# Attention and two MLPs in one kernel: the half tile of keys in the value product, high and low parts stacked on 128 partitions

## The chip, the cores and the metric

The kernel runs on one core of one Trainium2 chip. The metric is the device time of one execution in microseconds (us). All inputs and outputs are float32. Matrix products are made in the format fp32r, in which one pass of TensorE doesn't keep all the bits of a float32. So each float32 operand is split in two: a high part (the value rounded to fp32r) and a low part (the value minus its high part), and the products of the parts are added up in PSUM.

## The reference, cut to what matters

```
q, k, v: (4, 8, 576, 64)            # batch, heads, sequence, head dimension
q_rot, k_rot = rotate(q), rotate(k)
scores = matmul(q_rot, k_rot.T) / sqrt(64)
scores = scores - max(scores)       # over the keys
attn = exp(scores)
attn = attn / (sum(attn) + 1e-9)
x = matmul(attn, v)                 # the value product
x = x as (2304 tokens, 512)
x = (s * relu(x @ w_in)**2 + b) @ w_out       # first MLP, 512 -> 2048 -> 512
h = x @ w2_in
out = (h * sigmoid(1.702 * h)) @ w2_out       # second MLP
```

The change touches the last line of the attention, `matmul(attn, v)`.

## The kernel before

The 32 heads are worked off in 16 pairs, p = 0 to 15; the heads of a pair are h = 0 and h = 1. A head has 576 keys and 576 queries: four full tiles of 128 (NM = 4) and half a tile of 64 (TAIL = 64). The half tiles of the two heads of a pair share 128 partitions: the 64 keys of head 0 lie on partitions 0 to 63, those of head 1 on 64 to 127.

For each pair the kernel does these jobs, under short names that the prediction uses:

- **S** (TensorE, line 627; ST, line 642, for the half tiles): scores of one tile of 128 queries against all 576 keys, eight S jobs and one ST per pair.
- **max** (VectorE, lines 861 and 867) reads a score tile from PSUM and writes the negated row maximum; **exp** (ScalarE, lines 762 and 769) writes the exponentials E to SBUF, with an accumulator read behind each.
- **X, XQ, XT** (TensorE, lines 653, 663, 675 to 679): transposes, after which the keys lie on the partitions. XT makes the half tiles of keys of both heads, 128 partitions by 640 columns.
- **hi, hiQ, hiT** (ScalarE, lines 776, 781, 786) copy the transposed exponentials out of PSUM as high parts; **lo, loQ, loT** (VectorE, lines 871, 875, 879) subtract these from PSUM and leave the low parts. hiT and loT are for the half tiles of keys; each is one instruction of 128 partitions by 640 columns per pair.
- **V, vlo** (GpSimd, lines 540 and 544) split the value rows in a high and a low part, which stand side by side as the 128 stationary columns. The half tile of value rows is loaded on the 64 partitions of its own head, and the other 64 were set to zero once at the start (line 520), so that the keys of the other head count nothing.
- **PV0, PV1** (TensorE, line 699): the value product of head 0 and head 1. Over the five key tiles, the high and the low part of the exponentials pass in turn against the same stationary values. The output of 576 columns crosses a bank of PSUM, so a tile is done in two pieces (256 and 320 columns); the half tile of head 1 is done in three (256, 256 and 64), since its columns wrap around.
- **evac** (ScalarE, line 793) and **sum** (VectorE, line 891) copy the two halves of the output partitions out of PSUM (64 partitions by 576 columns each; sum moves its half to the other 64 partitions), and **finish** (GpSimd, lines 574 to 581) adds them and scales the result.
- **qk** and **klo** (lines 837 and 914) make high and low parts of the rotated queries and keys of a later pair from the transposes of **prep** (line 729).
- **icp** (line 798) copies the transposed reciprocals of the sums.

The order of the work is written out by hand, one list per engine. PE_ORDER, ACT_ORDER, DVE_ORDER, POOL_ORDER and SP_ORDER hold what one step of the loop issues, with a number behind @ that tells how many pairs a job is ahead or behind; the lists named FIRST do the start. Within one step the lists give, for the jobs around the change:

```
PE:   ... XQ XT X10 X11 IT X12 X13 S00 PV0 S01 S02 S03 ST S10 S11 S12 X00 X01 S13 PV1 prep0 ...
ACT:  ... evac1 qk0 hi02 qk1 hi03 hiQ hiT icp hi10 hi11 hi12 hi13 evac0 exp00 exp01 exp02 exp03 expT exp10 exp11 ...
DVE:  ... sum1 inv klo0 lo02 klo1 lo03 loQ loT lo10 lo11 lo12 lo13 max00 sum0 max01 max02 max03 maxT max10 ...
```

Jobs in PSUM take turns in its eight banks (SLOTS), and a job waits until the one before it in its banks has been read (`freed`, `read`). PV0 stands in the banks of XT, so it waits for loT twice over: for its operand and for its banks. S01 follows X11 and X13, S03 follows PV0, S10 follows S02, and PV1 follows S11. On SyncE, load_v (lines 465 and 466) issues two transfers per head for the value rows, behind a wait for vlo of the pair before (v_lo).

After pair 15, GpSimd does the last sums and splits for the first MLP, and both MLPs follow on all engines.

Of the kernel before, what the change touches and what calls it, by code (L numbers as in the profile page):

```python
# [10 lines left out]
P = 128  # L11


def need(eng, sem, value):

    if value > 0:
        eng.wait_ge(sem, value)
# [13 lines left out]
def fused_kernel(nc, q, k, v, w1_in, w1_out, w_s, w_b, w2_in, w2_out,  # L31
# [129 lines left out]
    with outer:  # L161
        def sem(name):
            return outer.enter_context(nc.semaphore(name))
# [53 lines left out]

        qk_in = [sem(f"qk_in{i}") for i in range(2)]
        v_in = [sem(f"v_in{i}") for i in range(2)]
        v_cleared = sem("v_cleared")  # L220
        cleared = sem("cleared")
        rot_step = sem("rot_step")
        rotated = sem("rotated")
# [46 lines left out]
        def read(eng, kind, p, h, j):  # L270
            if kind == "S":
                need(eng, exp_done, 2 * NM * p + NM * h + j + 1)
            elif kind == "ST":
                need(eng, expT_done, p + 1)
            elif kind == "X":
                need(eng, et_lo, 2 * NM * p + NM * h + j + 1)
            elif kind == "XQ":
                need(eng, etQ_lo, p + 1)
            elif kind == "XT":
                need(eng, etT_lo, p + 1)  # L280
            elif kind == "IT":
                need(eng, invT_copied, p + 1)
            elif kind == "PV":
                need(eng, evac_done, 2 * p + h + 1)
                need(eng, half_done, 2 * p + h + 1)
            elif kind == "prep":
                need(eng, qk_lo, 2 * p + h + 1)
# [44 lines left out]
        with ExitStack() as ctx:  # L332
# [25 lines left out]
            Xhi = sb("Xhi", [P, 2, NM, S], F32R)  # L358
            Xlo = sb("Xlo", [P, 2, NM, S], F32R)

            XThi = sb("XThi", [P, S + TAIL], F32R)
            XTlo = sb("XTlo", [P, S + TAIL], F32R)

            ET = [sb(f"ET{i}", [P, S + TAIL]) for i in range(2)]
            V = [sb(f"V{i}", [P, NT, 2, D], F32R) for i in range(2)]
# [79 lines left out]
            def attention_sync(sp):  # L445
                def tails(t, p):

                    return t[2 * p:2 * p + 2, MAIN:S, :]

                def load(p, h, _):  # L450

                    wait_rotated(sp, 2 * p - 2 + h)
                    to = group(raw, *HEAD_TILES[h])
                    for w, t in enumerate((q_h, k_h)):
                        sp.dma_start(to[:, w, 0:NM, :], mains(t, 2 * p + h)).then_inc(qk_in[h], 16)
                        if h == 0:
                            sp.dma_start(to[:, w, NM, :], tails(t, p)).then_inc(qk_in[h], 16)

                def load_next(p, h, _):
                    if p > 1:  # L460
                        load(p, h, 0)

                def load_v(p, h, _):
                    need(sp, v_lo, 2 * (p - 1) + h + 1)
                    sp.dma_start(vraw[:, h, 0:NM, :], mains(v_h, 2 * p + h)).then_inc(v_in[h], 16)
                    sp.dma_start(vraw[rows_of(h), h, NM, :], v_h[2 * p + h, MAIN:S, :]).then_inc(v_in[h], 16)

                def load_next_v(p, h, _):
                    if p > 0:
                        load_v(p, h, 0)  # L470


                def q_copies(p, h, _):
                    if p > 0:
                        sp.wait_ge(qk_lo, 2 * p + h + 1)
                        need(sp, s_done, 2 * NM * (p - 2) + NM * (h + 1))
                        need(sp, sT_done, p - 1)
                        at = h * TAIL
                        for part in range(2):
                            sp.dma_start(Q[h][p % 2][rows_of(part), at:at + S].bitcast(F32), QK[h][p % 2][0:D, part, :].bitcast(F32)).then_inc(q_copied[h], 16)  # L480

                def k_copy(p, h, _):
                    if p > 0:
                        sp.wait_ge(q_copied[h], 32 * p)
                        sp.dma_start(QK[h][p % 2][0:D, :, :].bitcast(F32), QK[h][p % 2][D:P, :, :].bitcast(F32)).then_inc(k_copied[h], 16)

                def put_inv(p, _, __):
                    sp.wait_ge(invT_copied, p + 1)
                    need(sp, inv_in[p % 2], 48 * (p // 2))
                    sp.dma_start(inv_dram[p % 2], invT[p % 2][:]).then_inc(inv_out[p % 2], 16)  # L490

                def get_inv(p, _, __):
                    sp.wait_ge(inv_out[p % 2], 16 * (p // 2 + 1))
                    need(sp, x_done, p)
                    flat = inv_dram[p % 2].rearrange("t p -> (t p)")
                    for h, at, a, n in ((0, 0, 0, S), (1, 0, S + TAIL, MAIN), (1, MAIN, S, TAIL)):
                        sp.dma_start(inv_row[rows_of(h), at:at + n],
                                     flat[a:a + n].rearrange("(o q) -> o q", o=1).to_broadcast([D, n])).then_inc(inv_in[p % 2], 16)

                def after(s):  # L500
                    if s in (6, 8):
                        load_win(sp, (6, 8).index(s))

                for w, t in enumerate((q_h, k_h)):
                    sp.dma_start(group(raw_0, 0, NM)[:, w, :, :], mains(t, 0)).then_inc(first_in[w], 16)
                for w, t in enumerate((q_h, k_h)):
                    sp.dma_start(group(raw_0, NM, NM + 1)[:, w, 0, :], tails(t, 0)).then_inc(first_tails_in, 16)
                for w, t in enumerate((q_h, k_h)):
                    sp.dma_start(group(raw_0, NM + 1, TILES)[:, w, :, :], mains(t, 1)).then_inc(first_in[2 + w], 16)
                load(1, 0, 0)  # L510
                load(1, 1, 0)
                sp.wait_ge(v_cleared, 1)
                load_v(0, 0, 0)
                load_v(0, 1, 0)
                sp.dma_start(sb_sb[:, 0:1], w_s.rearrange("(a b) -> a b", a=1).to_broadcast([P, 1])).then_inc(sb_in, 16)
                sp.dma_start(sb_sb[:, 1:2], w_b.rearrange("(a b) -> a b", a=1).to_broadcast([P, 1])).then_inc(sb_in, 16)
                program(SP_FIRST, SP_ORDER, {"load": load_next, "loadv": load_next_v, "qcopy": q_copies, "kcopy": k_copy, "put": put_inv, "get": get_inv}, after)

            def attention_gpsimd(pool):
                pool.memset(vraw[:, :, NM, :], 0.0).then_inc(v_cleared, 1)  # L520
                pool.memset(zero[:], 0.0)
                for i in range(2):
                    pool.memset(Q[0][i][:, S:NT * P].bitcast(F32), 0.0)
# [11 lines left out]
                        rotate(pool, g, byc, bys, rot_step, rotated, g - 2)  # L535

                def hi_V(p, h, _):
                    pool.wait_ge(v_in[h], 32 * (p + 1))
                    need(pool, pv_done, 2 * (p - 1) + h + 1)
                    pool.tensor_tensor(V[h][:, :, h, :], vraw[:, h, :, :], zero[:, :].unsqueeze(2).broadcast_to([P, NT, D]), ALU.add).then_inc(v_hi, 1)  # L540

# [68 lines left out]
            def attention_tensor(pe):  # L610
# [71 lines left out]
                def PV(p, h, _):  # L682
                    pe.wait_ge(v_lo, 2 * p + h + 1)
                    freed(pe, before[("PV", p, h, 0)])
                    pe.wait_ge(et_lo, 2 * NM * p + NM * (h + 1))
                    if h == 0:
                        pe.wait_ge(etQ_lo, p + 1)
                        pe.wait_ge(etT_lo, p + 1)
                    ps, r = banks("PV", p, h), ROW[0]
                    for j in range(NT):  # L690

                        pieces = PIECES[0] if j < NM or h == 0 else (PIECES[0][0], (BANK, r + MAIN, BANK - r), (r + MAIN, r + S, -TAIL))
                        for a, b, c in pieces:
                            for n in range(2):
                                if j < NM:
                                    x = (Xhi, Xlo)[n][:, h, j, c:c + b - a]
                                else:
                                    x = (XThi, XTlo)[n][:, TAIL + c:TAIL + c + b - a]
                                mm = pe.matmul(ps[:, a:b], V[h][:, j, :, :].rearrange("p a d -> p (a d)"), x,  # L699
                                               start=j == 0 and n == 0, stop=j == NM and n == 1, skip_group_check=True)  # L700
                    mm.then_inc(pv_done, 1)

                def rotated_tile(first, end, t, w):
# [43 lines left out]
            def attention_scalar(act):  # L747
# [35 lines left out]
                def hiT(p, _, __):  # L783
                    act.wait_ge(xT_t, p + 1)
                    need(act, pv_done, 2 * p)
                    act.copy(XThi[:], banks("XT", p)[:, ROW[1]:ROW[0] + S]).then_inc(etT_hi, 1)

                def evac(p, h, _):
                    act.wait_ge(pv_done, 2 * p + h + 1)
# [65 lines left out]
            def attention_vector(dve):  # L855
# [19 lines left out]
                    dve.tensor_tensor(Xlo[:, :, :, MAIN:S], by_heads(banks("XQ", p)), Xhi[:, :, :, MAIN:S].bitcast(F32), ALU.subtract).then_inc(etQ_lo, 1)  # L875

                def loT(p, _, __):
                    dve.wait_ge(etT_hi, p + 1)
                    dve.tensor_tensor(XTlo[:], banks("XT", p)[:, ROW[1]:ROW[0] + S], XThi[:].bitcast(F32), ALU.subtract).then_inc(etT_lo, 1)  # L879

                def invert(p, _, __):
                    dve.wait_ge(eps_done, p + 1)
# [523 lines left out]
```

## Time and profile before

| | before |
|---|---|
| median of 3 runs | 1085.67 us (1085.67 to 1087.19) |
| the profiled execution's own time | 1085.56 us |
| span of its profile | 1083.7 us |
| TensorE (PE) matmul busy | 1046.9 us, 97% |
| VectorE (DVE) busy | 733.1 us, 68% |
| ScalarE (ACT) busy | 634.0 us, 59% |
| GpSimd (POOL) busy | 706.8 us, 65% |
| mean granted TensorE clock | 0.995 of full |

The profiled execution takes 1.9 us more than its span, which lies around it. Its own time is 0.1 us below the median of the runs. The attention fills the first 320 us or so; the rest is the MLPs. The shares of busy time are means over both parts, which have different limits; PE's busy time counts each matmul until its modelled end, though the next one starts before that.

### The profile page before, as it was taken

The page shows a single profiled execution, that of the slowest core. Times are in us where ns is not written, and L with a number is a line of the kernel's source. Part 1 is how long each engine was busy: PE and PEld are TensorE (multiplying, and loading weights), DVE is VectorE, ACT ScalarE, POOL GpSimd, SP SyncE. Part 2 cuts the span into 40 slices and gives each one's busy share as a digit, 9 for nine tenths or more (in the row PEclk, how much of TensorE's full clock was granted, in tenths as well). Part 3 has the DMA queues.
Part 4 walks back from the last instruction along what each step waited for, and adds up shares of the span by engine and source line. Part 5 has one row for each costly group of instructions (what it writes and reads, how often), then busy time and mean ns, then how long its engine had stood idle before and what let it go on. Part 6 is the DMA issues. An engine that isn't in the chain of part 4 may idle for free.

```text
span 1083.7 us, 17067 instructions
## 1 busy us (share of the span) xinstructions
PE 1046.9 (97%) x6234; PEld 965.3 (89%) x6234; DVE 733.1 (68%) x874; ACT 634.0 (59%) x1124; POOL 706.8 (65%) x587
## 2 busy tenths in 40 slices
PE   4899999999978999999999999999999999999998
PEld 4899999999967999999999999999898888898987
DVE  6888888888857656766576654865567655854542
ACT  4887878787755445645555544754465445654442
POOL 6878787878679764676466665666656674565430
PEclk9999999999989999999999999999999999999999
DMA  4555455554113221222122212122221412142101
GB/s 112 128 149 152 110 148 142 153 128 124 42 49 98 88 68 59 78 60 78 60 63 73 79 59 78 59 73 64 75 62 54 141 59 78 59 136 59 59 21 58
DMA packets 100613, 93.03 MB, mean 86 GB/s; under 512 B 15652, under 2 KB 78644, under 8 KB 100532
## 3 DMA queue, kind: packets, MB, share of 16 engines
q1 hardware_dynamic: 99408, 90.94, 29.7%
q8 instruction: 50, 0.82, 0.3%
q10 hardware_dynamic: 1124, 1.02, 0.3%
q14 instruction: 31, 0.25, 0.1%
HBM read 69.44 MB, written 4.79 MB: 68 GB/s over the span
## 4 chain that ended last, share of the span: by engine, by line
PE 68%; POOL 1%; DVE 0%; issue 0%
PE psum L1106 37%; PE psum L1078 31%; POOL wout_lo L1033 0%; POOL win_lo L1023 0%; POOL wsum L1007 0%; POOL wsum L1009 0%; POOL wsum L1006 0%; POOL wsum L1011 0%; DVE x_sums L1135 0%; POOL xT L581 0%
## 5 line engine op out<-in xcount | busy, mean ns | idle before, releaser
L1023 POOL TENSOR_TENSOR win_lo<-win_raw,win_hi 128x768 fp32r<-128x768 f32 x48 | 101.0, 2104 | 249.0 <-ACT win_hi L1017 249.0
L1078 PE MATMUL psum<-xc_hi,win_hi 128*128 128x384 f32 x672 | 227.0, 338 | 7.7 <-POOL xc_lo L558 4.0
L1078 PE MATMUL psum<-xc_lo,win_hi 128*128 128x384 f32 x672 | 226.8, 338 | 0.0
L1078 PE MATMUL psum<-xc_hi,win_lo 128*128 128x384 f32 x672 | 226.3, 337 | 0.0
L1078 PEld LDWEIGHTS psum<-xc_hi,win_hi 128*128 128x128 f32 x672 | 127.0, 189 | 17.4 <-POOL xc_lo L558 4.4
L1078 PEld LDWEIGHTS psum<-xc_lo,win_hi 128*128 128x128 f32 x672 | 126.9, 189 | 8.2
L1033 POOL TENSOR_TENSOR wout_lo<-wout_raw,wout_hi 128x1024 fp32r<-128x1024 f32 x48 | 119.8, 2495 | 16.5 <-ACT wout_hi L1235 16.5
L1078 PEld LDWEIGHTS psum<-xc_hi,win_lo 128*128 128x128 f32 x672 | 126.9, 189 | 0.0
L762 ACT ACTIVATE E<-psum,negmax 128x576 f32<-128x576 f32 x128 | 94.7, 745 | 13.1 <-DVE negmax L861 13.0
L861 DVE TENSOR_REDUCE negmax<-psum 128x1 f32<-128x576 f32 x128 | 90.9, 751 | 14.2 <-PE psum L627 13.6
L1027 DVE TENSOR_TENSOR win_lo<-wsum,win_hi 128x1024 fp32r<-128x1024 f32 x47 | 96.6, 2056 | 4.3 <-ACT win_hi L1017 4.1
L1279 DVE TENSOR_TENSOR h_b<-psum,P 128x384 f32<-128x384 f32 x48 | 26.7, 556 | 104.1 <-PE psum L1078 104.1
L627 PE MATMUL psum<-QK,Q 128*128 128x320 f32 (+1 forms) x512 | 86.1, 309 | 9.2 <-ACT E L762 6.7
L871 DVE TENSOR_TENSOR Xlo<-psum,Xhi 128x512 fp32r<-128x512 f32 x128 | 82.6, 680 | 4.6 <-ACT Xhi L776 4.5
L627 PEld LDWEIGHTS psum<-QK,Q 128*128 128x128 f32 x512 | 71.8, 191 | 14.0 <-issue 6.8
L1283 DVE TENSOR_TENSOR h_a<-psum,U 128x384 f32<-128x384 f32 x48 | 26.7, 557 | 82.6 <-PE psum L1078 82.6
L1006 POOL TENSOR_TENSOR wsum<-win_raw 128x256 f32<-128x256 f32 x48 | 63.8, 1329 | 20.2 <-DVE win_lo L1027 18.8
L699 PE MATMUL psum<-Xhi,V 128*128 128x256 f32 (+1 forms) x256 | 71.3, 306 | 0.5 <-DVE XTlo L879 0.5
L653 PE MATMUL psum<-id_sb,E 128*128 128x128 f32 x512 | 70.2, 276 | 0.8 <-DVE Xlo L871 0.4
L699 PE MATMUL psum<-Xlo,V 128*128 128x256 f32 (+1 forms) x256 | 70.4, 299 | 0.0
L776 ACT CAST Xhi<-psum 128x512 fp32r<-128x512 f32 x128 | 69.3, 582 | 0.3 <-PE psum L653 0.2
L1235 ACT CAST wout_hi<-wout_raw 128x1024 fp32r<-128x1024 f32 x48 | 50.6, 1054 | 28.3 <-PE psum L1106 26.8
(154 smaller groups left out, 2849.2 us busy)
## 6 DMA issues: line engine op xcount, KB each, us to landing
wout_raw<-in_moe_w_out_dram SPq DMA_DIRECT2D x48, 512.0 KB, 3.6
win_raw<-in_moe_w_in_dram SPq DMA_DIRECT2D x48, 256.0 KB, 2.8
win_raw<-in_moe_w_in_dram SPq DMA_DIRECT2D x96, 128.0 KB, 2.8
Q<-QK SPq DMA_DIRECT2D x60, 144.0 KB, 2.8
QK<-QK SPq DMA_DIRECT2D x30, 288.0 KB, 3.4
vraw<-in_v_dram SPq DMA_DIRECT2D x32, 128.0 KB, 2.5
raw<-in_q_dram SPq DMA_DIRECT2D x30, 128.0 KB, 2.9
raw<-in_k_dram SPq DMA_DIRECT2D x30, 128.0 KB, 2.8
```

What stands on the lines that cost most here:

```text
L627: mm = pe.matmul(ps[:, a:b], Q[h][p % 2][:, at:at + P], QK[h][p % 2][:, part, c:c + b - a], start=part == 0, stop=part == 1)
L653: mm = pe.transpose(ps[:, t * P:(t + 1) * P], E[p % 2][:, t, h, c:c + P], id_sb[:])
L699: mm = pe.matmul(ps[:, a:b], V[h][:, j, :, :].rearrange("p a d -> p (a d)"), x, start=j == 0 and n == 0, stop=j == NM and n == 1, skip_gro ...
L762: act.activation(E[p % 2][:, j, h, :], row(banks("S", p, h, j), h), ACT.Exp, bias=negmax[p % 2][:, c:c + 1], accum_out=sums[p % 2][:, c:c ...
L776: act.copy(Xhi[:, h, j, 0:MAIN], banks("X", p, h, j)).then_inc(et_hi, 1)
L861: dve.tensor_reduce(negmax[p % 2][:, c:c + 1], row(banks("S", p, h, j), h), AX_X, ALU.max, negate=True).then_inc(max_done, 1)
L871: dve.tensor_tensor(Xlo[:, h, j, 0:MAIN], banks("X", p, h, j), Xhi[:, h, j, 0:MAIN].bitcast(F32), ALU.subtract).then_inc(et_lo, 1)
L1023: pool.tensor_tensor(win_lo[m % 2][:, 0:3 * BLK], win_raw[m % 2][:, 0:3 * BLK], win_hi[m % 2][:, 0:3 * BLK].bitcast(F32), ALU.subtract).th ...
L1027: last = eng.tensor_tensor(win_lo[m % 2][:, 3 * BLK:7 * BLK], wsum[:], win_hi[m % 2][:, 3 * BLK:7 * BLK].bitcast(F32), ALU.subtract)
L1033: pool.tensor_tensor(wout_lo[m % 2][:], wout_raw[m % 2][:], wout_hi[m % 2][:].bitcast(F32), ALU.subtract).then_inc(wout_lo_done, 1)
L1078: mm = pe.matmul(hps(n, k), w[n % 2][:, at:at + P], x[k][:, t, :], start=k in FRESH and t == 0 and i == 0, stop=t == HK - 1 and i == 2, sk ...
L1106: mm = pe.matmul(yps(bank)[:, col:col + size], lhsT, rhs, start=first and col == 0 and i == 0, stop=last and i == 2, skip_group_check=True)
```

## The change

The half tile of exponentials of each head gets a buffer of its own, XC0 and XC1, on 128 partitions. The high part stays on the partitions of its head, and the low part is written to the other 64. The half tile of value rows is loaded twice, onto both halves of the partitions, and the clearing at the start is dropped. The value product of the half tile is then one pass over XC in place of one over XThi and one over XTlo. hiT and loT become two instructions each, of 64 partitions by 576 columns, and each signals for itself; what takes the banks of XT waits for both.

```diff
@@ read
             elif kind == "XT":
-                need(eng, etT_lo, p + 1)
+                need(eng, etT_lo, 2 * p + 2)
@@ buffers
-            XThi = sb("XThi", [P, S + TAIL], F32R)
-            XTlo = sb("XTlo", [P, S + TAIL], F32R)
+            XC = [sb(f"XC{h}", [P, S + TAIL], F32R) for h in range(2)]
@@ load_v
-                    sp.dma_start(vraw[rows_of(h), h, NM, :], v_h[2 * p + h, MAIN:S, :]).then_inc(v_in[h], 16)
+                    for half in range(2):
+                        sp.dma_start(vraw[rows_of(half), h, NM, :], v_h[2 * p + h, MAIN:S, :]).then_inc(v_in[h], 16)
@@ attention_sync
-                sp.wait_ge(v_cleared, 1)
@@ attention_gpsimd
-                pool.memset(vraw[:, :, NM, :], 0.0).then_inc(v_cleared, 1)
@@ hi_V
-                    pool.wait_ge(v_in[h], 32 * (p + 1))
+                    pool.wait_ge(v_in[h], 48 * (p + 1))
@@ PV
+                    pe.wait_ge(etT_lo, 2 * p + h + 1)
                     if h == 0:
                         pe.wait_ge(etQ_lo, p + 1)
-                        pe.wait_ge(etT_lo, p + 1)
                     ps, r = banks("PV", p, h), ROW[0]
-                    for j in range(NT):
-
-                        pieces = PIECES[0] if j < NM or h == 0 else (PIECES[0][0], (BANK, r + MAIN, BANK - r), (r + MAIN, r + S, -TAIL))
-                        for a, b, c in pieces:
-                            for n in range(2):
-                                if j < NM:
-                                    x = (Xhi, Xlo)[n][:, h, j, c:c + b - a]
-                                else:
-                                    x = (XThi, XTlo)[n][:, TAIL + c:TAIL + c + b - a]
-                                mm = pe.matmul(ps[:, a:b], V[h][:, j, :, :].rearrange("p a d -> p (a d)"), x,
-                                               start=j == 0 and n == 0, stop=j == NM and n == 1, skip_group_check=True)
+                    for j in range(NM):
+                        for a, b, c in PIECES[0]:
+                            for n, x in enumerate((Xhi, Xlo)):
+                                pe.matmul(ps[:, a:b], V[h][:, j, :, :].rearrange("p a d -> p (a d)"), x[:, h, j, c:c + b - a],
+                                          start=j == 0 and n == 0, stop=False, skip_group_check=True)
+
+                    for a, b, c in (PIECES[0] if h == 0 else ((r, BANK, TAIL), (BANK, r + MAIN, TAIL + BANK - r), (r + MAIN, r + S, 0))):
+                        mm = pe.matmul(ps[:, a:b], V[h][:, NM, :, :].rearrange("p a d -> p (a d)"), XC[h][:, c:c + b - a],
+                                       start=False, stop=True, skip_group_check=True)
@@ hiT
-                    act.copy(XThi[:], banks("XT", p)[:, ROW[1]:ROW[0] + S]).then_inc(etT_hi, 1)
+                    for h in range(2):
+                        act.copy(XC[h][rows_of(h), 0:S], row(banks("XT", p), h)[rows_of(h), :]).then_inc(etT_hi, 1)
@@ loT
-                    dve.wait_ge(etT_hi, p + 1)
-                    dve.tensor_tensor(XTlo[:], banks("XT", p)[:, ROW[1]:ROW[0] + S], XThi[:].bitcast(F32), ALU.subtract).then_inc(etT_lo, 1)
+                    for h in range(2):
+                        dve.wait_ge(etT_hi, 2 * p + h + 1)
+                        dve.tensor_tensor(XC[h][rows_of(1 - h), 0:S], row(banks("XT", p), h)[rows_of(h), :],
+                                          XC[h][rows_of(h), 0:S].bitcast(F32), ALU.subtract).then_inc(etT_lo, 1)
```

## Rows read from the trace of the kernel before

**Rows 1.** Busy time by stretch: us, engines busy (x instructions), granted clock, DMA share, GB/s.
```profile
201.98:220.12 18.14, 17.75 (x141) 16.78 (x139) 15.82 (x24) 14.57 (x33) 14.89 (x16) 1.00 0.53 135
...
25.00:30.00 5.00, 3.73 (x25) 3.26 (x25) 3.45 (x5) 3.56 (x8) 4.78 (x6) 1.00 0.58 139
```

**Rows 2.** Waits from 60 to 360 us: total us, times, longest.
```profile
PE psum L627 <- ACT E L762: 5.2, 13, 0.6
```

**Rows 3.** TensorE in one pair: start us, us, instruction, count [idle before <- releaser].
```profile
207.87 0.31 PE L699 MATMUL psum<-Xhi,V 128*128 128x256 f32 x1
...
210.03 0.28 PE L699 MATMUL psum<-XThi,V 128*128 128x256 f32 x1
...
210.57 1.87 PE L627 MATMUL psum<-QK,Q 128*128 128x256 f32 x12
...
214.05 1.82 PE L627 MATMUL psum<-QK,Q 128*128 128x320 f32 x12 [0.39 <-ACT E L762]
...
217.29 0.35 PE L699 MATMUL psum<-Xhi,V 128*128 128x256 f32 x1
...
219.49 0.28 PE L699 MATMUL psum<-XThi,V 128*128 128x256 f32 x1
...
220.11 0.33 PE L727 MATMUL psum<-id_sb,rot 128*128 128x128 f32 x1
```

**Rows 4.** VectorE in the same pair.
```profile
203.62 0.82 DVE L914 SCALAR_TENSOR_TENSOR QK<-psum,qk_scale,QK 128x576 fp32r<-128x576 f32 x1 [0.45 <-ACT QK L837]
...
206.27 0.68 DVE L875 TENSOR_TENSOR Xlo<-psum,Xhi 128x512 fp32r<-128x512 f32 x1
206.87 0.81 DVE L879 TENSOR_TENSOR XTlo<-psum,XThi 128x640 fp32r<-128x640 f32 x1
207.60 2.47 DVE L871 TENSOR_TENSOR Xlo<-psum,Xhi 128x512 fp32r<-128x512 f32 x4
209.99 0.74 DVE L861 TENSOR_REDUCE negmax<-psum 128x1 f32<-128x576 f32 x1
210.77 0.76 DVE L891 COPY osum<-psum 64x576 f32<-64x576 f32 x1
211.56 2.09 DVE L861 TENSOR_REDUCE negmax<-psum 128x1 f32<-128x576 f32 x3
...
220.32 0.75 DVE L891 COPY osum<-psum 64x576 f32<-64x576 f32 x1 [0.71 <-PE psum L699]
```

**Rows 5.** ScalarE in the same pair.
```profile
205.52 0.74 ACT L786 CAST XThi<-psum 128x640 fp32r<-128x640 f32 x1
...
206.78 2.00 ACT L776 CAST Xhi<-psum 128x512 fp32r<-128x512 f32 x4
210.77 0.63 ACT L793 COPY O<-psum 64x576 f32<-64x576 f32 x1 [1.99 <-PE psum L699]
...
212.35 0.74 ACT L762 ACTIVATE E<-psum,negmax 128x576 f32<-128x576 f32 x1 [0.22 <-DVE negmax L861]
...
213.08 0.73 ACT L762 ACTIVATE E<-psum,negmax 128x576 f32<-128x576 f32 x1
```

**Rows 6.** The value tile: DMA issue on SyncE's queue, ns min/median/max.
```profile
L466 SPq DMA_DIRECT2D vraw<-in_v_dram x32: 471/524/1503, 9.8 to 299.4; - x32
```

**Rows 7.** What SyncE's queue waited for, 60 to 310 us.
```profile
SPq L465 <- POOL V L544: 48.2, 12, 9.5
```

**Rows 8.** TensorE and VectorE in the first pairs.
```profile
39.72 0.27 PE L742 MATMUL psum<-id_sb,inv 128*9 128x128 f32 x1 [0.53 <-ACT E L762]
...
45.18 0.76 DVE L891 COPY osum<-psum 64x576 f32<-64x576 f32 x1 [0.61 <-PE psum L699]
```

**Rows 9.** GpSimd at the end of the attention, first and last of 21 rows.
```profile
291.47 0.72 POOL L540 TENSOR_TENSOR V<-vraw,zero 128x320 fp32r<-128x320 f32 x1 [4.18 <-PE psum L699]
...
317.50 0.73 POOL L1011 TENSOR_TENSOR wsum<-win_raw,wsum 128x256 f32<-128x256 f32 x1
```

**Rows 10.** ScalarE behind it.
```profile
318.34 0.83 ACT L1016 CAST win_hi<-win_raw 128x768 fp32r<-128x768 f32 x1 [8.91 <-POOL wsum L1011]
```

More of the change, by code:

```diff
@@ L219, in fused_kernel @@
         v_in = [sem(f"v_in{i}") for i in range(2)]
-        v_cleared = sem("v_cleared")
         cleared = sem("cleared")
```

## The prediction

> **What bounds the kernel now.** I read the busy time by stretch first. In one steady pair, from the end of one PV1 to the end of the next (18.14 us), TensorE is busy 17.75 us and VectorE 15.82 us [rows 1]. That looks like a bound by TensorE with 2.3 us of room on VectorE, and it would make the change pay. Next come the waits: TensorE stood idle for exp, before S10, 13 times for 5.2 us in all, so about once per pair [rows 2]. An engine that waits once per pair isn't the whole bound; a chain through the others closes the loop. The timelines of one pair show that chain, followed back from the wait:
>
> - S10 starts at 214.05 after 0.39 us idle for exp02 [rows 3]. exp02 (213.08) follows exp01 without a gap, and exp01 (212.35) waited 0.22 us for max01 [rows 5].
> - On VectorE, max01 (211.56) follows sum0 (210.77), max00 (209.99), four lo (207.60), loT (206.87), loQ (206.27), and so on without idle time back to klo0 at 203.62, which waited for ScalarE's qk, which comes behind PV1 of the pair before [rows 4].
> - PV0 (207.87) starts 0.19 us after loT has ended (206.87 + 0.81 = 207.68) [rows 3, 4]. evac0 sits idle 1.99 us and starts at 210.77, the moment PV0 is done, and so does sum0 [rows 4, 5]. The two branches behind loT, one through PV0 and one through VectorE's own queue, thus meet at sum0 with no room on either: max00 ends at 210.73.
>
> So the reader should see that VectorE is full from klo0 to max01 though its share over the pair is 87%, that its 2.3 us of idle time lie elsewhere (0.71 us of them before sum1 [rows 4]), and that loT is on the chain that sets the pair's period. TensorE's share from S10 to the end of PV1 is on it too: 214.05 to 220.11, back to back [rows 3].
>
> **What the change removes.** The tail of PV0, four matmuls, takes 210.57 - 210.03 = 0.54 us, that of PV1, six, 220.11 - 219.49 = 0.62 us [rows 3]. One pass in place of two leaves half: 0.27 us saved in PV0. In PV1 the three passes left take between 0.27 us (half a pair of 64 columns included) and 0.35 us; I take 0.32, so 0.30 saved. Together 0.57 us of TensorE per pair, 9.1 us over 16 pairs. What is on the chain is PV1's 0.30; PV0's 0.27 lies on the branch that gets room (below) and is worth nothing.
>
> **What it adds on VectorE.** loT of 640 columns becomes two of 576, on 64 partitions each. A copy of 64 partitions by 576 columns takes 0.76 us, as long as a reduction of 128 by 576 (0.74) [rows 4], so half the partitions save no time. No row has a subtraction of 576 columns: between 512 (0.68) and 640 (0.81) lies 0.745, and klo with 576 columns and a scale takes 0.82 [rows 4]. I take 0.745, the upper bound is 0.82. Now the gaps. Neighbours that stay on the same partitions overlap: loT starts 0.08 us before loQ has ended, and the first lo starts 0.08 before loT has ended. The sum copy, which writes the other 64 partitions, doesn't: it starts 0.04 after max00 has ended, and max01 starts 0.03 after sum0 has ended [rows 4]. The new loT instructions also write to the other half, and the first lo behind them goes back. If all three are held as the copy is, loQ to the first lo becomes 206.95 + 0.03 + 0.745 + 0.03 + 0.745 + 0.03 = 208.53 in place of 207.60: **+0.93 us per pair**. With full overlap it would be 2 x 0.665 - 0.73 = +0.60; with 0.82 each and no overlap +1.08.
>
> The Trainium skill, VectorE: DVE Perf Modes, section Two Vector instructions with no wait between them, says that an instruction is held until all earlier ones have finished if an input or the output starts in another group of 32 partitions than the last one in that memory. The rows above agree for the copy; for a subtraction no row here shows it. By that rule all three starts are held, the +0.93; without it +0.60.
>
> **On ScalarE**, hiT (0.74) becomes two copies like evac, 0.63 each [rows 5]: +0.53 at most. The second is done near 205.52 + 2 x 0.63 = 206.78, before the second loT would start (207.76), and the four hi behind it move to about 207.3, still ahead of the lo at 208.53. ScalarE then idles 1.99 us before evac0, which takes the rest in. Nothing on the chain. Without that cover it would be 0.53 per pair.
>
> **The sum along both branches of a pair.** VectorE's branch: sum0 and max01 +0.93. PV0's branch: second loT ends at 208.50, +0.82, less 0.27, so PV0's end is +0.55, less than 0.93 and hidden. S01 waits for the last lo (+0.93, to about 211.1), close to when PV0 ends (211.3), and S03 waits for sum0; both stay ahead of VectorE, which reaches max03 two reductions later. So exp01, exp02 and S10 are +0.93, and PV1 ends at 0.93 - 0.30 = **+0.63 us**. The other branch, TensorE's own 17.75 us less 0.57, is far below 18.77.
>
> **Transfers.** 32 more, one per head, each some 0.5 us of issue on SyncE (median 524 ns) [rows 6], about 1 us per pair. SyncE waited 48.2 us in 12 waits before the value loads alone [rows 7], so this delays only what it would have waited for. Taken as 0; the upper bound, were a load late every pair, is 1.0. The wait dropped at the start and the 128 columns not cleared: 0.
>
> **Over the kernel.** In pair 0 the first IT waits for an exp that stands behind a max behind loT, and VectorE had 0.61 us idle before sum0 [rows 8]: two longer loT against two shorter PV, about 0. Pairs 1 to 13 each give +0.63, the last a little less (its prep is gone): 12 x 0.63 + 0.55 = 8.1 us. From PV1 of pair 13 on, GpSimd works without a gap from 291.47 to 318.2, 21 instructions, and ScalarE waits 8.91 us for it [rows 9, 10]. Everything behind that keeps its distance; the changes in pairs 14 and 15 are hidden under it, and the MLPs aren't touched. The profiled execution, 1085.56, would come to 1093.7; the median of the runs is 0.1 us higher: **1093.8 us**.
>
> **Rivals.**
> - *TensorE bounds after all (faster).* The 0.57 us per pair count in full and VectorE takes the longer loT into its 2.3 us: 16 x 0.57 = 9.1 us off, 1076.6. For it: 97% busy. Against it: the wait before S10 in every pair, and no idle time between loT and max01. It decides if loT costs the chain less than 0.30 us per pair; all bounds above give 0.60 or more. 0.10, with the cases between.
> - *No hold.* loT adds 0.60, so 0.30 net per pair, 13 x 0.30 = 3.9 us, 1089.6. For it: the subtractions overlap today [rows 4]. Against: the copy doesn't. 0.15.
> - *No change.* Some 0.3 us per pair of VectorE time come back through the order of waits, for instance because S01 to S03 start earlier against max. 1085.7 to 1087.8. 0.06.
> - *More than forecast.* Subtractions of 0.82 us, or SyncE's queue late: (1.08 - 0.30) x 13 = 10.1 us, 1095.8, with the transfers up to 1108. 0.07.
> - *TensorE's clock falls.* It would now idle some 1.6 us per pair. In a stretch of 5 us with 3.73 busy the granted clock was 1.00, the upper of its two levels [rows 1]. Under 0.02, within the last rival.
>
> **The numbers.** 0.62 for the forecast, its own range 1091.5 to 1096. A measurement of this kernel can tell 0.2%, 2.2 us, from no change. Faster 0.10, within 0.2% 0.06, slower 0.84. The range takes in the missing hold and the upper bound of the subtraction: 1088.5 to 1097.5.
>
> **What the profile would show.** Right: 32 VectorE subtractions of 64x576 near 0.75 us in place of 16 of 128x640; from the point where loT starts now (206.87) 1.66 us to the first lo, not 0.73; TensorE idle about 0.8 us before PV0 for XC, and still idle for exp before S10; the pair's period 18.77, not 18.14; 80 tail matmuls in place of 160; GpSimd's run to the end of the attention starting near 299.6. Wrong: a period under 18.14 with no wait before PV0, or a first lo that overlaps the second loT.

## The result and the profile after

The changed kernel takes 1094.59 us (median of 4 runs, 1094.53 to 1095.67) against 1086.43 us for the kernel before beside it: a ratio of 1.0074, with a 95% interval of 1.0061 to 1.0087. It is slower, by about 8 us. The forecast was 1093.8 us, slower by 8.1.

The page of the changed kernel, two lines of it:

```profile
span 1092.8 us, 16984 instructions
...
PE 1043.2 (95%) x6154; PEld 956.2 (88%) x6154; DVE 747.1 (68%) x890; ACT 642.5 (59%) x1140; POOL 706.1 (65%) x586
```

TensorE has 80 matmuls and 3.7 us of busy time less, VectorE has 16 instructions and 14.0 us more, and the span is 9.1 us longer. TensorE's share fell from 97% to 95%: it was relieved of work, and its idle time grew by 12.8 us.

One steady pair on TensorE, as rows 3 show it of before:

```profile
214.63 0.36 PE L690 MATMUL psum<-Xhi,V 128*128 128x256 f32 x1 [0.59 <-DVE XC L876]
...
216.83 0.43 PE L694 MATMUL psum<-XC,V 128*128 128x256 f32 x2
217.10 1.33 PE L624 MATMUL psum<-QK,Q 128*128 128x256 f32 x8
218.64 0.77 PE L624 MATMUL psum<-QK,Q 128*128 128x256 f32 x4 [0.22 <-DVE osum L889]
...
221.02 1.18 PE L624 MATMUL psum<-QK,Q 128*128 128x320 f32 x7 [0.45 <-ACT E L757]
```

The tail of PV0 now takes 217.10 - 216.83 = 0.27 us, half of before. Against that stand three waits in the pair: 0.59 us before PV0 for the new loT, 0.22 us before S03 for sum0, and the 0.45 us before S10 for exp02, which was 0.39. The first two are new. The same pair on VectorE, to be held against rows 4:

```profile
212.27 0.68 DVE L871 TENSOR_TENSOR Xlo<-psum,Xhi 128x512 fp32r<-128x512 f32 x1
212.99 1.54 DVE L876 TENSOR_TENSOR XC<-psum,XC 64x576 fp32r<-64x576 f32 x2
214.56 2.48 DVE L867 TENSOR_TENSOR Xlo<-psum,Xhi 128x512 fp32r<-128x512 f32 x4
...
217.74 0.76 DVE L889 COPY osum<-psum 64x576 f32<-64x576 f32 x1
```

From loQ to the first lo it is 214.56 - 212.27 = 2.29 us; it was 207.60 - 206.27 = 1.33. So loT costs 0.96 us more. The first loT starts 0.04 us after loQ has ended (212.95), and the first lo 0.03 us after the second loT has (214.53): no overlap at either end.

Which of the two branches behind loT ends last is read at sum0 (217.74 above) and evac0, the ScalarE copy right behind PV0:

```profile
216.96 0.75 DVE L857 TENSOR_REDUCE negmax<-psum 128x1 f32<-128x576 f32 x1
```

```profile
217.29 0.63 ACT L789 COPY O<-psum 64x576 f32<-64x576 f32 x1 [2.28 <-PE psum L694]
```

PV0 is done at 217.29. sum0, which reads the same output, starts only at 217.74, right behind max00 (ended at 217.71). VectorE's branch is now the later one by 0.45 us; before, both met at 210.77.

The pair's period is read from evac1, the ScalarE copy right behind PV1, here of pair 2 and of pair 12 in the changed kernel:

```profile
95.67 0.63 ACT L789 COPY O<-psum 64x576 f32<-64x576 f32 x1 [0.36 <-PE psum L694]
...
283.18 0.64 ACT L789 COPY O<-psum 64x576 f32<-64x576 f32 x1 [0.35 <-PE psum L694]
```

That is 187.51 us for ten pairs, a period of 18.75 us. In the kernel before it is 18.15 us:

```profile
93.27 0.64 ACT L793 COPY O<-psum 64x576 f32<-64x576 f32 x1 [0.68 <-PE psum L699]
...
274.72 0.64 ACT L793 COPY O<-psum 64x576 f32<-64x576 f32 x1 [0.68 <-PE psum L699]
```

And at the end of the attention, GpSimd:

```profile
300.44 0.72 POOL L537 TENSOR_TENSOR V<-vraw,zero 128x320 fp32r<-128x320 f32 x1 [4.75 <-PE psum L694]
...
326.36 0.73 POOL L1009 TENSOR_TENSOR wsum<-win_raw,wsum 128x256 f32<-128x256 f32 x1
```

Its run of 21 instructions starts 8.97 us later than before [rows 9] and ends 8.86 us later; the span is longer by 9.1. So all but 0.2 us of the loss is there when the attention ends, and the MLPs add next to nothing in this profile.

### The profile page after: what moved, and what is told of

The parts are those of the page before. It is cut to its first block, busy times and chain, and to the rows that moved or that the text cites. A ratio compares the mean times of both kernels' runs of the same rounds, so it can differ in the third digit from the quotient of the medians.

```text
span 1092.8 us, 16984 instructions
## 1 busy us (share of the span) xinstructions
PE 1043.2 (95%) x6154; PEld 956.2 (88%) x6154; DVE 747.1 (68%) x890; ACT 642.5 (59%) x1140; POOL 706.1 (65%) x586
## 4 chain that ended last, share of the span: by engine, by line
PE 68%; POOL 1%; DVE 0%; issue 0%
PE psum L1104 37%; PE psum L1076 31%; POOL wout_lo L1031 0%; POOL win_lo L1021 0%; POOL wsum L1005 0%; POOL wsum L1007 0%; POOL wsum L1004 0%; POOL wsum L1009 0%; DVE x_sums L1133 0%; POOL xT L578 0%
## 5 line engine op out<-in xcount | busy, mean ns | idle before, releaser
L624 PE MATMUL psum<-QK,Q 128*128 128x320 f32 (+1 forms) x512 | 89.4, 312 | 12.9 <-ACT E L757 7.5
```

Of the source, the lines that this page charges most:

```text
L624: mm = pe.matmul(ps[:, a:b], Q[h][p % 2][:, at:at + P], QK[h][p % 2][:, part, c:c + b - a], start=part == 0, stop=part == 1)
```

## The experiments

Each kernel was compared with the kernel before on the same chip. Periods are measured as above, from evac1 of pair 2 to that of pair 12, divided by ten.

| kernel | ratio to before | 95% interval | period, us | against 18.15 |
|---|---|---|---|---|
| changed | 1.0074 | 1.0061 to 1.0087 | 18.75 | +0.61 |
| pv0_once | 0.9991 | 0.9982 to 1.0001 | 18.14 | -0.01 |
| pv1_once | 0.9962 | 0.9949 to 0.9975 | 17.79 | -0.35 |
| v_twice | 0.9998 | 0.9989 to 1.0008 | 18.15 | 0.00 |
| hi_split | 1.0024 | 1.0014 to 1.0033 | 18.18 | +0.04 |
| split64 | 1.0102 | 1.0088 to 1.0116 | 18.99 | +0.85 |
| two128 | 1.0071 | 1.0056 to 1.0087 | 18.74 | +0.60 |
| skip_lo1 | 0.9985 | 0.9976 to 0.9994 | 17.97 | -0.18 |
| dma_stack | 0.9962 | 0.9950 to 0.9975 | 17.79 | -0.36 |
| after_again | 1.0056 | 1.0039 to 1.0073 | 18.76 | +0.62 |
| before_again | 1.0000 | 0.9990 to 1.0009 | 18.15 | 0.00 |

### What TensorE's saving is worth: pv0_once and pv1_once

The edit, for head 0 (pv1_once has 1 for 0):

```diff
-                            for n in range(2):
+                            for n in range(1 if j == NM and h == 0 else 2):
```

> The kernel before with the tail of PV0 passed once (the low part of the half tile is left out for head 0): 0.27 us less of TensorE per pair, nothing added on VectorE. If the chain runs klo0 - loT - max01 - exp02 - S10 - PV1 on VectorE, that time lies on a branch with room and is worth nothing: 0 to -0.1 us per pair, 1085 to 1086.5, period 18.1 us. If TensorE's own time is the bound, 16 x 0.27 = 4.3 us off.

> The same for PV1 (the low part of the half tile is left out for head 1): 0.30 us less of TensorE per pair. Both theories give the same here, since PV1 closes the chain: period 17.84 us, 13 to 16 x 0.30 = 3.9 to 4.8 us off. Less than 2 us off would say that something beside PV1 sets the period too.

TensorE saves nearly the same in both, 0.27 us of work in PV0 and 0.34 in PV1, and the two kernels come out apart: 0.01 us per pair for PV0, 0.35 for PV1. In pv0_once, PV0 is done earlier and nothing follows from it:

```profile
209.74 0.75 DVE L861 TENSOR_REDUCE negmax<-psum 128x1 f32<-128x576 f32 x1
210.52 0.76 DVE L891 COPY osum<-psum 64x576 f32<-64x576 f32 x1
...
213.80 1.82 PE L627 MATMUL psum<-QK,Q 128*128 128x320 f32 x12 [0.46 <-ACT E L762]
```

PV0's last matmul is followed by S01 at 210.04, but sum0 starts at 210.52, when VectorE has ended max00, and the wait before S10 grows from 0.39 to 0.46 us. This is what "beside the chain" looks like: the saved time turns up as waiting. If TensorE were the bound, pv0_once would have been 4.3 us faster; its interval ends at 2 us.

### What the longer loT costs, and why: split64 and two128

split64 splits hiT and loT in two halves of the partitions that stay where they are; TensorE's work is the same as before. Like hi_split below, it also clears XThi and XTlo once at the start, on GpSimd. The part on loT:

```diff
-                    dve.wait_ge(etT_hi, p + 1)
-                    dve.tensor_tensor(XTlo[:], banks("XT", p)[:, ROW[1]:ROW[0] + S], XThi[:].bitcast(F32), ALU.subtract).then_inc(etT_lo, 1)
+                    for h in range(2):
+                        dve.wait_ge(etT_hi, 2 * p + h + 1)
+                        dve.tensor_tensor(XTlo[rows_of(h), TAIL * (1 - h):TAIL * (1 - h) + S], row(banks("XT", p), h)[rows_of(h), :],
+                                          XThi[rows_of(h), TAIL * (1 - h):TAIL * (1 - h) + S].bitcast(F32), ALU.subtract).then_inc(etT_lo, 1)
```

> The kernel before with hiT and loT both split in two instructions of 64 partitions by 576 columns that stay on their own partitions; TensorE's work is unchanged. The added VectorE time alone. Second loT and first lo start behind the end of the one before (held), the first loT overlaps: +0.85 us per pair on the chain, period 19.0 us, 1096.5 to 1098. If TensorE were the bound, 2.3 us of room on VectorE would take it: 1086. If half the partitions cost half the time: no change.

two128 has two loT of 576 columns as well, but on all partitions:

```diff
-                    dve.tensor_tensor(XTlo[:], banks("XT", p)[:, ROW[1]:ROW[0] + S], XThi[:].bitcast(F32), ALU.subtract).then_inc(etT_lo, 1)
+                    for c, to in ((TAIL, XTlo), (0, XTlo1)):
+                        dve.tensor_tensor(to[:, c:c + S], banks("XT", p)[:, ROW[1] + c:ROW[1] + c + S], XThi[:, c:c + S].bitcast(F32), ALU.subtract).then_inc(etT_lo, 1)
```

> The kernel before with loT done in two instructions of all 128 partitions by 576 columns (head 1 reads its low part from the second one's tile). Same columns as in the changed kernel, but no change of partitions. If only a change of partitions keeps neighbours from overlapping: +0.60 to 0.65 us per pair, period 18.75 to 18.8, 1094, and every one of these starts 0.08 us before the one ahead has ended. If each extra instruction costs the full gap, the same as the split in halves, period 19.0.

Both landed on the first theory: +0.85 and +0.60 us per pair. The rows tell why they differ. split64 first:

```profile
213.84 0.68 DVE L878 TENSOR_TENSOR Xlo<-psum,Xhi 128x512 fp32r<-128x512 f32 x1
214.43 1.53 DVE L883 TENSOR_TENSOR XTlo<-psum,XThi 64x576 fp32r<-64x576 f32 x2
216.00 2.48 DVE L874 TENSOR_TENSOR Xlo<-psum,Xhi 128x512 fp32r<-128x512 f32 x4
```

and two128:

```profile
213.19 0.68 DVE L876 TENSOR_TENSOR Xlo<-psum,Xhi 128x512 fp32r<-128x512 f32 x1
213.79 1.41 DVE L881 TENSOR_TENSOR XTlo<-psum,XThi 128x576 fp32r<-128x576 f32 x2
215.12 2.47 DVE L872 TENSOR_TENSOR Xlo<-psum,Xhi 128x512 fp32r<-128x512 f32 x4
```

In two128 each start comes 0.08 us before the end of the one ahead (213.79 against 213.87, 215.12 against 215.20), and the pair of loT takes 1.41 us. One of them takes 0.746 us in the median, on 128 partitions; in split64, on 64 partitions, it is 0.755. In split64 the first loT, which begins on partition 0 as loQ did, still overlaps (214.43 against 214.52); the two take 1.53 us, and the first lo, back from partition 64 to 0, starts 0.04 after their end. In the changed kernel the first loT doesn't overlap either, because it writes to partitions 64 to 127. So from loQ to the first lo: 1.33 us before, 1.93 in two128, 2.16 in split64, 2.29 in the changed kernel. Of the added 0.96 us, 0.60 are the second instruction's columns and 0.36 the three lost overlaps.

By the rule of the Trainium skill (VectorE: DVE Perf Modes, Two Vector instructions with no wait between them), the first loT of split64 isn't held, the second and the first lo are, and none is in two128. The traces agree at each of these starts, now for subtractions too.

### The parts beside VectorE: hi_split and v_twice

hi_split is the kernel before with only hiT in two copies (and the clearing of XThi and XTlo at the start); v_twice has only the 32 added transfers, into a spare tile, and V waits for them. The part on the transfers:

```diff
-                    sp.dma_start(vraw[rows_of(h), h, NM, :], v_h[2 * p + h, MAIN:S, :]).then_inc(v_in[h], 16)
+                    for to in (vraw[rows_of(h), h, NM, :], vspare[rows_of(1 - h), h, :]):
+                        sp.dma_start(to, v_h[2 * p + h, MAIN:S, :]).then_inc(v_in[h], 16)
```

> The kernel before with ScalarE's hiT split in two copies of 64 partitions by 576 columns, loT as it was behind both: +0.53 us of ScalarE per pair. My theory: loT starts up to 0.1 us later at most, 0 to +1.3 us over the kernel. If ScalarE's part of the change is on the chain: +0.5 us per pair, 7 us more.

> The kernel before with each half tile of value rows transferred a second time, to a spare tile, and waited for: the 32 added transfers alone. My theory: 0, SyncE has room. Rival: the 1.0 to 1.6 us by which the changed kernel lost more than the pairs explain (its first transposes start 0.6 us later, and the granted clock falls to half between 25 and 29 us) comes from these transfers at the start; then this kernel is 1 to 1.6 us slower and shows the same fall of the clock.

The transfers cost nothing. The split of hiT cost 0.04 us in a steady pair, as expected, but 1.0024 over the kernel, 2.6 us, which is a miss: 1.3 was the most I had expected. Two rows of ScalarE in hi_split, evac1 of pair 0 and evac0 of pair 1, show the largest part of it that belongs to the split:

```profile
56.49 0.64 ACT L796 COPY O<-psum 64x576 f32<-64x576 f32 x1 [0.66 <-PE psum L701]
...
65.83 0.63 ACT L796 COPY O<-psum 64x576 f32<-64x576 f32 x1 [1.51 <-PE psum L701]
```

They lie 9.34 us apart, and 8.86 in the kernel before (55.88 and 64.74): in pair 1, whose order is another one, ScalarE's hiT is on the chain with nearly its whole 0.5 us. Another 0.31 us come in pair 13 (16.95 us from evac1 of pair 12 to that of pair 13, before 16.64). With 0.04 in each of the ten pairs between, the split is worth 1.2 us.

In the changed kernel the stretch in pair 1 is 9.55 us, 0.69 more than before, which is loT's 0.96 less PV0's 0.27: nothing is left over for ScalarE. In skip_lo1 (next), where VectorE has less to do, it is 9.09 us, 0.23 more, though PV0 is 0.27 shorter. So VectorE's longer time covers this cost in the changed kernel.

Beside it, TensorE's clock fell in this kernel's profile: at the start (below), and once in the first MLP, where TensorE works without idle time:

```profile
342.00:346.00 4.00, 4.00 (x17) 3.72 (x16) 3.04 (x2) 1.40 (x3) 4.00 (x2) 0.57 0.63 210
```

The granted clock is 0.57 there, and 1.00 in the kernel before. The 24 matmuls from 340.95 to 346.78 take 5.83 us, and the same ones 4.30 in the kernel before (339.13 to 343.43), so this fall alone costs the profiled execution 1.53 us. How often it falls there in other executions isn't on record.

### The changed kernel without one loT: skip_lo1

```diff
-                    for h in range(2):
-                        dve.wait_ge(etT_hi, 2 * p + h + 1)
+                    for h in range(1):
+                        dve.wait_ge(etT_hi, 2 * p + 2)
```

> The changed kernel without the second loT (the low part of the half tile is left out for head 1; its place holds zeros). VectorE's chain keeps one subtraction of 576 columns with a held start on both sides: 0.17 us more than in the kernel before, less 0.30 for PV1: -0.13 us per pair, period 18.0, 1084 to 1085.5. If the change's loss came from the doubled ScalarE copies, the transfers or the waits and not from VectorE, it would stay near 1094.

Here the low part of head 1 is left out, and XC1 is cleared once at the start. The period falls from 18.75 to 17.97 us, though both copies of ScalarE, all transfers and the single pass are still there. One VectorE subtraction with its gaps is thus worth 0.78 us per pair, its own duration (0.756 in the median of the changed kernel) and 0.03. What VectorE has more than before is 0.16 us, from loQ to the first lo (205.05 to 206.54, 1.49 against 1.33). The kernel is as much faster than before as PV1's saving exceeds that: 0.35 - 0.16 = 0.19 per pair by the rows, 0.18 by the period.

### A version that beats both: dma_stack

Since of the two savings only PV1's counts, and of the added work it is VectorE's that hurts, head 1 alone is stacked, and a transfer does it. The tail keys of head 0 keep their two passes. On SyncE, between put and get, and on TensorE:

```diff
+                def x_copy(p, _, __):
+                    sp.wait_ge(pv_done, 2 * p + 1)
+                    sp.wait_ge(etT_lo, p + 1)
+                    sp.dma_start(XThi[0:D, 0:S].bitcast(F32), XTlo[D:P, 0:S].bitcast(F32)).then_inc(xt_copied, 16)
...
+                        if j == NM and h == 1:
+                            pe.wait_ge(xt_copied, 16 * (p + 1))
...
-                            for n in range(2):
+                            for n in range(1 if j == NM and h == 1 else 2):
```

The half tile of value rows is loaded on both halves for head 1 only.

> The kernel before, whole computation, in which only head 1 is stacked, and by a transfer: hiT and loT stay single; once PV0 is done, SyncE copies head 1's low half tile over head 0's high part (64 partitions by 576 columns), its value rows are loaded on both halves, and PV1's tail takes one pass. VectorE has nothing added, PV1 0.30 us less, and the copy lands some 3 us after its issue near 0.1 us behind PV0, about 9 us ahead of PV1's tail: period 17.84, 3.9 us off over 13 pairs, 1081.5 to 1083. If the copy or SyncE's queue is late, TensorE shows a wait before the tail of PV1 and the gain is gone.

The whole computation in 0.9962 of the time before (interval 0.9950 to 0.9975), about 4 us less, and about 12 less than the changed kernel. The rows of one pair, SyncE's queue, then TensorE:

```profile
207.78 0.47 SPq L505 DMA_DIRECT2D XThi<-XTlo  x1
```

```profile
214.34 0.35 PE L708 MATMUL psum<-Xhi,V 128*128 128x256 f32 x1
...
216.53 0.43 PE L708 MATMUL psum<-XThi,V 128*128 128x256 f32 x3
216.81 0.32 PE L736 MATMUL psum<-id_sb,rot 128*128 128x128 f32 x1
```

The transfer is issued at 207.78, right behind PV0 (S01 starts at 207.58). These 16 transfers land a median 2.3 us after issue, so this one near 210.1, 6.4 us before PV1's tail at 216.53. The tail takes 0.28 us without a wait. It was 0.62. The period is 17.79 us, the same as in pv1_once, where the low part is left out: the transfer is fully hidden.

### The start: after_again and before_again

> The changed kernel once more, for its start. In its first profile TensorE began at 11.48 us (before: 10.86) and its granted clock fell to half between 25 and 29 us, about 1 us together that the sum over pairs does not hold. If these vary from one execution to the next and are no part of the change: a steady period of 18.75 us again, but another start, and maybe no fall. If they belong to the change: 11.5 us and the fall again.

> The kernel before once more, for the same question: period 18.14 us. If start and fall vary by themselves, the start may lie anywhere between 10.8 and 12.1 us, as in the other profiles of kernels whose start is the same, and its time spreads by some 0.2%. If they belong to the change: 10.9 us and no fall. Ratio 1.000.

The first row is the changed kernel's first profile, and below it are after_again's and before_again's first matmul:

```profile
25.00:30.00 5.00, 4.46 (x22) 3.92 (x22) 3.36 (x5) 3.11 (x9) 4.78 (x6) 0.66 0.51 123
```

```profile
11.75 0.45 PE L709 MATMUL psum<-id_sb,E 128*128 128x128 f32 x1 [11.75 <-POOL E L440]
```

```profile
11.21 0.45 PE L714 MATMUL psum<-id_sb,E 128*128 128x128 f32 x1 [11.21 <-POOL E L442]
```

The mean granted clock between 25 and 30 us is 0.66: for part of the stretch TensorE had the lower of its two levels, 1.2 GHz. It is 0.66 in after_again too, and 1.00 in before_again as in rows 1. So the fall came back with the changed kernel. It isn't the change's alone: hi_split has 0.69 and two128 0.66 there, while split64, v_twice, skip_lo1, pv0_once, pv1_once and dma_stack have 1.00. The transfers don't bring it (v_twice), and neither does the first matmul's time: 10.61 us in hi_split, 12.06 in two128, 11.23 in split64. What decides it stays open; that the clearing at the start is dropped was not tested by itself. The start itself does vary from profile to profile, 10.86 and 11.21 us in two of the same kernel.

What the fall costs can be read between two fixed points of TensorE's order, the first four transposes of the scores behind a wait for exp and the eight S matmuls behind a later one. Before:

```profile
22.55 0.63 PE L653 MATMUL psum<-id_sb,E 128*128 128x128 f32 x4 [0.34 <-ACT E L762]
...
31.07 1.39 PE L627 MATMUL psum<-QK,Q 128*128 128x256 f32 x8 [1.22 <-ACT E L762]
```

and in the changed kernel:

```profile
23.02 0.63 PE L650 MATMUL psum<-id_sb,E 128*128 128x128 f32 x4 [0.34 <-ACT E L757]
...
32.06 1.36 PE L624 MATMUL psum<-QK,Q 128*128 128x256 f32 x8 [1.21 <-ACT E L757]
```

They are 8.52 us apart before (8.52 in before_again, 8.48 in split64) and 9.04 in the changed kernel (9.12 in after_again, 9.03 in hi_split, 9.13 in two128). The fall costs 0.5 to 0.6 us.

## Why the prediction was right, step by step

- **The chain.** That the pair's period is set by VectorE from klo0 to max01, then exp02, S10 and PV1, was right. skip_lo1 and split64 move the period by the VectorE time taken or added, and pv0_once by 0.01 us. The rival in which TensorE bounds is out: it was busy for 17.75 us of 18.14, and that was no bound.
- **The removed passes.** PV0's 0.27 us: measured 0.27, worth 0.01, forecast 0. PV1's: forecast 0.30, measured 0.62 - 0.28 = 0.34 by the rows and 0.35 by the period. My 0.32 us for the three passes left was too high; they take 0.28.
- **The longer loT.** Forecast +0.93, measured +0.96. A subtraction of 64 by 576 takes 0.756 us, not the 0.745 read between its neighbours; on 128 partitions and without the hold, in two128, it takes 0.746. The rival without the hold (+0.60) is what two128 shows when no instruction changes partitions; the changed kernel isn't that case.
- **The sum per pair.** +0.63 forecast, +0.61 measured; both small errors nearly cancel. The period was to be 18.77 and is 18.75.
- **ScalarE and the transfers.** "Nothing on the chain" holds in a steady pair (0.04 and 0.00 us). For ScalarE it is wrong in pairs 1 and 13, where hi_split shows 0.48 and 0.31 us; in the changed kernel VectorE's longer time covers that in pair 1, and pair 13 comes out as the sum had it.
- **The pairs at the start.** Forecast: pair 0 gives about 0 and pair 1 and 2 give 1.26, so +1.26 us at evac1 of pair 2. Measured: 95.67 - 93.27 = +2.40. Of the missing 1.14 us, 0.47 are a later start (0.62 at the first matmul, 11.48 against 10.86; 0.47 at the transposes, 23.02 against 22.55), part of which varies between profiles, and 0.52 the fall of the clock, by the rows above. Neither was in my sum. The last 0.15 us stay open. I gave the clock rival under 0.02 and looked for it in the steady pairs, where the clock is 1.00; it fell at the start instead.
- **The end.** +0.51 us from pair 12 to pair 13 (forecast 0.55), and then nearly a fixed distance, 8.97 us later at the start of GpSimd's run and 9.1 at the end of the span: right.
- **The waits foretold.** TensorE idles 0.59 us before PV0, not 0.8, since a wait is counted from the modelled end of the matmul ahead. For S03 the prediction had the wait for sum0 but no time. It is 0.22 us, and it is hidden: VectorE goes from sum0 through max01, max02 and max03 to maxT (217.74 to 220.61) without a gap.

That the total of 8.1 us was hit so closely is partly luck. The profile lost 9.1 us, 1.0 more than the sum, while the medians moved by 8.2 in the first comparison and 6.2 in the second (1093.42 against 1087.25; interval 4.2 to 7.9 us, just short of 8.1). The medians of the kernel before in the comparisons lay between 1086.4 and 1087.4, all above the 1085.67 from which I started, and its runs between 1085.4 and 1088.7. So the last one or two microseconds aren't settled. The periods, which repeat to about 0.01 us between profiles of the same kernel, carry the finding: 12 pairs of 0.61 and 0.51 in pair 13 make 7.8 us.

## What to carry to other kernels

Before halving an engine's work, follow the wait that recurs once per round back to the instruction it stands on, and see whether the work lies in front of it or beside it: here two savings of nearly the same size on a 97% busy engine, 0.34 and 0.27 us, were worth 0.35 and 0.01 us per pair. Rearranging operands for TensorE is paid by whoever writes them; on VectorE a subtraction of 576 columns took 0.755 us on half the partitions and 0.746 on all, and each change of partitions between neighbours cost 0.12 us more. When the rearranged operand isn't needed at once, a transfer can do it on queues that have room: here it landed 6.4 us ahead of its use.

## What I had not expected of the hardware

TensorE's granted clock fell between 25 and 30 us to a mean of 0.66 to 0.69 in four profiles of three kernels (changed, hi_split, two128), with 4.2 to 4.6 of 5 us busy, and stayed at 1.00 in the same stretch of kernels that have the same work there in the same order (3.61 to 3.73 of 5 us busy in both profiles of the kernel before and in split64). The higher busy time is the slower matmuls: the eight S matmuls at 25.02 take 1.32 us before, and those at 25.49 in the changed kernel 2.07. In the steady pairs, where the changed kernel idles in three places, it never fell.

Around the end of the attention it fell in all twelve profiles, for some microseconds between 302 and 346 us, and not at the same place in two profiles of one kernel: at about 312 to 320 and 324 to 327 us in one of the kernel before, at about 316 to 320 and 333 to 337 in the other. In nine profiles this left the time from GpSimd's last split of the attention's end to the end of the span at 766.2 to 766.5 us. In pv0_once, pv1_once and hi_split, where a fall came more than 20 us behind that split, it was 767.8 to 769.0. So up to 2.8 us of a profile's span can have nothing to do with the pairs, and the periods compare better. What decides where the clock falls stays open.
